# First products of the second MLP moved to the output's banks, P2 ahead of P6, and the last unit taken by halves

## What is computed

```python
x = attention(q, k, v)                 # 2 x 768 tokens, 8 heads of 64; local window and block means
# first MLP, 512 -> 1536 -> 512
rms = sqrt(mean(x * x, axis=-1) + 1e-6)
xn = x / rms * rms_g
g = xn @ w_gate
x = (g * sigmoid(g) * (xn @ w_val)) @ w_out
# second MLP, 512 -> 2048 -> 512
h = x @ w_in2
out = (h - tanh(h)) @ w_out2
```

## Time and profile before

| | |
|---|---|
| median of 3 runs | 623.73 us (623.37 to 624.0) |
| profiled execution, its own time | 624.17 us |
| its span in the trace | 622.0 us |
| PE busy | 610.6 us (98%) |
| DVE, ACT, POOL busy | 429.9, 323.8, 171.1 us |
| TensorE clock granted | 9 of 10 or more in every slice of the page |

### The profile page before, as it was taken

How to read it: one execution, slowest core, us unless ns; L and a number is a source line. 1 busy time by engine, 2 the same in 40 slices (tenths; PEclk the granted TensorE clock), 3 DMA queues, 4 the chain that set the end, 5 groups by cost and what they waited for, 6 DMA issues and landing times.

```text
span 622.0 us, 10724 instructions
## 1 busy us (share of the span) xinstructions
PE 610.6 (98%) x3990; PEld 569.2 (92%) x3990; DVE 429.9 (69%) x699; ACT 323.8 (52%) x622; POOL 171.1 (28%) x223
## 2 busy tenths in 40 slices
PE   8989999999999999999999999999999999999997
PEld 7669999999999998889898899999999989888986
DVE  4899777766653659877776789999534496666643
ACT  5676545444433337555555567766333275555542
POOL 4675421202110322222220745561200222222200
PEclk9999999999999999999999999999999999999999
DMA  9999722332211303222221342224123032222102
GB/s 255 193 241 221 144 63 66 94 94 41 80 53 51 87 9 89 81 69 68 69 69 34 106 134 69 67 69 122 49 76 94 0 99 73 68 69 69 34 2 101
DMA packets 96186, 53.90 MB, mean 87 GB/s; under 512 B 33736, under 2 KB 90312, under 8 KB 95944
## 3 DMA queue, kind: packets, MB, share of 16 engines
q1 hardware_dynamic: 95704, 52.44, 32.6%
q10 hardware_dynamic: 432, 0.79, 0.3%
HBM read 50.07 MB, written 3.15 MB: 86 GB/s over the span
## 4 chain that ended last, share of the span: by engine, by line
PE 90%; ACT 4%; DVE 3%; POOL 2%; issue 1%; DVEq 0%; POOLq 0%; ACTq 0%
PE bank L938 11%; PE bank L940 11%; PE bank L942 11%; PE bank L881 10%; PE bank L883 10%; PE bank L882 10%; PE bank L1047 7%; PE bank L1046 7%; PE bank L1045 7%; PE bank L845 1%; PE bank L865 1%; PE bank L815 1%; POOL sm L614 1%; ACT kT L1224 1%; PE bank L740 1%
## 5 line engine op out<-in xcount | busy, mean ns | idle before, releaser
L1712 DVE TENSOR_TENSOR h_lo<-pd,h_hi 128x384 fp32r<-128x384 f32 x112 | 71.9, 643 | 28.9 <-ACT h_hi L1438 14.0
L1047 PE MATMUL bank<-y_hi,h_lo 128*128 128x512 f32 x192 | 75.5, 393 | 0.0
L1046 PE MATMUL bank<-y_lo,h_hi 128*128 128x512 f32 x192 | 75.4, 393 | 0.0
L1045 PE MATMUL bank<-y_hi,h_hi 128*128 128x512 f32 x192 | 75.3, 392 | 0.0
L704 POOL TENSOR_TENSOR ws_raw<-x_raw 128x256 f32<-128x256 f32 x16 | 11.9, 746 | 209.2 <-PE bank L942 127.6
L881 PE MATMUL bank<-h_hi,z_hi 128*128 128x384 f32 x192 | 64.9, 338 | 0.0
L883 PE MATMUL bank<-h_hi,z_lo 128*128 128x384 f32 x192 | 64.5, 336 | 0.0
L882 PE MATMUL bank<-h_lo,z_hi 128*128 128x384 f32 x192 | 64.5, 336 | 0.0
L1305 ACT CAST h_hi<-pd 128x384 fp32r<-128x384 f32 x48 | 24.7, 515 | 45.5 <-DVE pd L1742 33.5
L1422 ACT COPY part<-bank 128x384 f32<-128x384 f32 x48 | 22.9, 478 | 43.4 <-PE bank L942 42.2
L1047 PEld LDWEIGHTS bank<-y_hi,h_lo 128*128 128x128 f32 x192 | 36.0, 188 | 8.2
(11 more groups left out here) (207 smaller groups left out, 1721.9 us busy)
## 6 DMA issues: line engine op xcount, KB each, us to landing
x_raw<-in_moe_w_in_dram SPq DMA_DIRECT2D x32, 256.0 KB, 3.3
y_raw<-in_moe_w_out_dram SPq DMA_DIRECT2D x32, 256.0 KB, 2.8
x_raw<-in_moe_w_gate_dram SPq DMA_DIRECT2D x24, 256.0 KB, 3.2
y_raw<-in_moe_w_val_dram SPq DMA_DIRECT2D x24, 256.0 KB, 3.3
z_raw<-in_moe_w_out_dram SPq DMA_DIRECT2D x16, 384.0 KB, 3.3
k_rows<-in_k_dram SPq DMA_DIRECT2D x8, 384.0 KB, 5.7
qn<-in_q_dram SPq DMA_DIRECT2D x12, 256.0 KB, 6.6
vw_early<-in_v_dram SPq DMA_DIRECT2D x12, 192.0 KB, 6.3
```

The source lines that it names most:

```text
L1045: nc.tensor.matmul(AB[t][:], a_hi, w_hi, start=begins, stop=False, skip_group_check=True)
L1046: nc.tensor.matmul(AB[t][:], a_hi, w_lo, start=False, stop=False, skip_group_check=True)
L1047: last = nc.tensor.matmul(AB[t][:], a_lo, w_hi, start=False, stop=ends, skip_group_check=True)
L1712: nc.vector.tensor_tensor(dst, full, high.bitcast(f32), ALU.subtract).then_inc(done, 1)
```

## The change

`first_pair` gets banks of its own, all among the six of the output: P1, P6, P7, P4 in bank 7 (`UB0`), P5 in bank 4 (`VB0`, as before), P2 in bank 5 (`WB0`), P3 in bank 6 (`ZB0`). The waits follow: P1 of the next pair no longer waits for the difference of C21, nor its P2 for the sum C12, and the units that begin banks 4 to 7 wait for the readers of those banks instead. P3 no longer waits for the sum C11. `ORDER0`, and the code with it, has the second row of P2 ahead of the second row of P6.

The last unit of all is taken by halves of its columns: DVE first copies the right half of bank 7 (all but the last unit's share) to `stage` (`tail_kept`); PE adds the left half to bank 7 and computes the right half alone into bank 0, three matmuls of 256 columns each; DVE copies the left half and adds bank 0 to the kept right half.

```diff
-        UB, VB, VB0 = bank[0][:, 0:NB], bank[1][:, 0:NB], bank[4][:, 0:NB]
+        UB, VB = bank[0][:, 0:NB], bank[1][:, 0:NB]
+
+        UB0, VB0, WB0, ZB0 = bank[7][:, 0:NB], bank[4][:, 0:NB], bank[5][:, 0:NB], bank[6][:, 0:NB]
...
-        ORDER0 = ("P1", "P5", "P6", "P2", "P7", "P3", "P4")
+        ORDER0 = ("P1", "P5", "P2", "P6", "P7", "P3", "P4")
...
+        def chain_bank(p):
+            return UB if p % NP else UB0
...
                 if begins and t == 2:
-                    pe.wait_ge(total_done, total_no(p, "C12a"))
+                    pe.wait_ge(total_done, total_no(p, "C22"))
+                if begins and t == 3:
+                    pe.wait_ge(total_done, total_no(p, "C11"))
+                if begins and t == 4:
+                    pe.wait_ge(total_done, total_no(p, "C12"))
+                if begins and t == 5:
+                    pe.wait_ge(diff_done, tile_no(p, "C21"))
...
+                if p == G * NP - 1 and k == len(UNITS) - 1:
+
+                    half = DM // 2
+                    pe.wait_ge(diff_done, tile_no(p, "C21"))
+                    pe.wait_ge(tail_kept, 1)
+                    nc.tensor.matmul(AB[t][:, 0:half], a_hi, w_hi[:, 0:half], start=False, stop=False,
+                                     skip_group_check=True)
...
+                    nc.tensor.matmul(bank[0][:, 0:half], a_hi, w_hi[:, half:DM], start=True, stop=False)
...
             def first_pair(g):
                 p = g * NP
                 pe.wait_ge(x_lo_done, pair_weight(p, 0) + 1)
-                pe.wait_ge(x2_dve, x2_dve_no(g, 3))
-                quarter(UB, *operands(p, "P1"), start=True).then_inc(quarter_mm, 1)
-                pe.wait_ge(ws_lo_done, p + 1)
+                pe.wait_ge(x2_dve, x2_dve_no(g, KH))
                 if g:
                     pe.wait_ge(out_act, TT // 2)
                     pe.wait_ge(out_dve, TT // 2)
                 else:
                     pe.wait_ge(xT_lo_done, NT)
+                quarter(UB0, *operands(p, "P1"), start=True).then_inc(quarter_mm, 1)
+                pe.wait_ge(ws_lo_done, p + 1)
                 quarter(VB0, *operands(p, "P5"), start=True).then_inc(quarter_mm, 1)
-                quarter(VB, *operands(p, "P2"), start=True, rows=(0,))
+                pe.wait_ge(x2_dve, x2_dve_no(g, KC - 1))
+                quarter(WB0, *operands(p, "P2"), start=True, rows=(0,))
                 pe.wait_ge(part_done, 3 * p + 1)
-                quarter(UB, *operands(p, "P6"), rows=(0,))
-                pe.wait_ge(x2_dve, x2_dve_no(g, 3) + 5)
-                quarter(UB, *operands(p, "P6"), rows=(1,)).then_inc(quarter_mm, 1)
-                quarter(VB, *operands(p, "P2"), rows=(1,)).then_inc(quarter_mm, 1)
-                pe.wait_ge(x2_dve, x2_dve_no(g, 3) + 6)
+                quarter(UB0, *operands(p, "P6"), rows=(0,))
+                pe.wait_ge(x2_dve, x2_dve_no(g, KC - 1) + 1)
+                quarter(WB0, *operands(p, "P2"), rows=(1,)).then_inc(quarter_mm, 1)
+                pe.wait_ge(x2_dve, x2_dve_no(g, KC - 1) + 5)
+                quarter(UB0, *operands(p, "P6"), rows=(1,)).then_inc(quarter_mm, 1)
+                pe.wait_ge(x2_dve, x2_dve_no(g, KC - 1) + 6)
                 pe.wait_ge(part_done, 3 * p + 2)
-                quarter(UB, *operands(p, "P7")).then_inc(quarter_mm, 1)
+                quarter(UB0, *operands(p, "P7")).then_inc(quarter_mm, 1)
...
-                pe.wait_ge(total_done, total_no(p, "C11"))
-                quarter(VB, *operands(p, "P3"), start=True).then_inc(quarter_mm, 1)
+                quarter(ZB0, *operands(p, "P3"), start=True).then_inc(quarter_mm, 1)
...
             def next_pair(g, i):
...
-                pe.wait_ge(diff_done, tile_no(p - 1, "C21"))
+                if i > 1:
+                    pe.wait_ge(diff_done, tile_no(p - 1, "C21"))
                 quarter(UB, *operands(p, "P1"), start=True).then_inc(quarter_mm, 1)
                 units(1 if i == 1 else 2)
-                pe.wait_ge(total_done, total_no(p - 1, "C12"))
+                if i > 1:
+                    pe.wait_ge(total_done, total_no(p - 1, "C12"))
                 quarter(VB, *operands(p, "P2"), start=True).then_inc(quarter_mm, 1)
...
+                    if g + 1 == G and t == TT - 3:
+
+                        nc.vector.tensor_copy(stage[:, TT - 1, DM // 2:DM],
+                                              AB[TT - 1][:, DM // 2:DM]).then_inc(tail_kept, 1)
...
-                        for c0 in (0, DM // 2):
-                            nc.vector.tensor_copy(stage[:, t, c0:c0 + DM // 2],
-                                                  AB[t][:, c0:c0 + DM // 2]).then_inc(out_dve, 1)
+                        half = DM // 2
+                        nc.vector.tensor_copy(stage[:, t, 0:half], AB[t][:, 0:half]).then_inc(out_dve, 1)
+                        dve.wait_ge(tail_kept, 1)
+                        dve.wait_ge(w2_mm, NP * (g + 1))
+                        nc.vector.tensor_tensor(stage[:, t, half:DM], stage[:, t, half:DM], bank[0][:, 0:half],
+                                                ALU.add).then_inc(out_dve, 1)
```

More of the change, by code:

```diff
@@ L1044, in down_unit @@
                 a_hi, a_lo = h2_hi[:, s, row, b, c0:c0 + P], h2_lo[:, s, row, b, c0:c0 + P]
+                if p == G * NP - 1 and k == len(UNITS) - 1:
[4 more added lines that the diff above has]
+                                     skip_group_check=True)
+                    nc.tensor.matmul(AB[t][:, 0:half], a_hi, w_lo[:, 0:half], start=False, stop=False,
+                                     skip_group_check=True)
+                    nc.tensor.matmul(AB[t][:, 0:half], a_lo, w_hi[:, 0:half], start=False, stop=True,
+                                     skip_group_check=True).then_inc(acc_mm, 1)
+                    nc.tensor.matmul(bank[0][:, 0:half], a_hi, w_hi[:, half:DM], start=True, stop=False)
+                    nc.tensor.matmul(bank[0][:, 0:half], a_hi, w_lo[:, half:DM], start=False, stop=False)
+                    nc.tensor.matmul(bank[0][:, 0:half], a_lo, w_hi[:, half:DM], start=False,
+                                     stop=True).then_inc(w2_mm, 1)
+                    return
                 nc.tensor.matmul(AB[t][:], a_hi, w_hi, start=begins, stop=False, skip_group_check=True)
@@ L1421, in keep_part @@
                 act.wait_ge(quarter_mm, quarter_no(p, product))
-                nc.scalar.copy(part[:, k, :], UB).then_inc(part_done, 1)
+                nc.scalar.copy(part[:, k, :], chain_bank(p)).then_inc(part_done, 1)
             def tanh_tile(p, name):
@@ L1427, in tanh_tile @@
                     act.wait_ge(quarter_mm, quarter_no(p, "P4"))
-                    src = UB
+                    src = chain_bank(p)
                 else:
@@ L1911, in diff_tile @@
                 no = tile_no(p, name) - 1
-                src = UB if name == "C21" else total[:, TOTALS.index(name), :]
+                src = chain_bank(p) if name == "C21" else total[:, TOTALS.index(name), :]
                 dve.wait_ge(tanh2_done, no + 1)
@@ L1926, in first_pair @@
                 x2_bottom(g, KC - 1)
-                add_total(p, "C11", "P2", 3 * p + 1, part[:, 0, :], VB)
+                add_total(p, "C11", "P2", 3 * p + 1, part[:, 0, :], WB0)
                 add_total(p, "C12a", "P5", 3 * p + 2, part[:, 1, :], VB0)
@@ L1933, in first_pair @@
                 dve.wait_ge(total_done, total_no(p, "C12a"))
-                add_total(p, "C12", "P3", 3 * p + 2, total[:, TOTALS.index("C12"), :], VB)
+                add_total(p, "C12", "P3", 3 * p + 2, total[:, TOTALS.index("C12"), :], ZB0)
                 diff_tile(p, "C22")
@@ L2129, in _ @@
                         split_up_sums(0, GATE)
-                    if t < TT - 1:
+                    if g + 1 < G and t == TT - 1:
+                        dve.wait_ge(w2_mm, NP * (g + 1))
+                    else:
                         dve.wait_ge(acc_mm, (TT - 1) * g + t + 1)
-                    else:
-                        dve.wait_ge(w2_mm, NP * (g + 1))
                     if g:
                         dve.wait_ge(out_sent, 16 * TT * g)
+                    if g + 1 == G and t == TT - 3:
+                        nc.vector.tensor_copy(stage[:, TT - 1, DM // 2:DM],
+                                              AB[TT - 1][:, DM // 2:DM]).then_inc(tail_kept, 1)
                     if g + 1 < G or t < TT - 1:
```

9 lines of the change are left out of this document (5 added, 4 removed).

## The result

The changed kernel takes **625.21 us** (median of 10 runs, 624.4 to 626.66); the kernel before, run beside it, 623.94 (10 runs, 623.34 to 624.47). The ratio is 1.0017, with a 95% interval of 1.0009 to 1.0025: 1.06 us longer, between 0.56 and 1.56 (the two medians as they stand lie 1.27 apart). That is surely slower. By the 0.2% of the prediction it counts as no change, but only just: the interval reaches beyond 0.2%. The profiled execution took 625.03 us with a span of 623.3.

The account below looks back on a forecast made before the run. PE was taken as the bound, busy 610.6 of 622.0 us. Group 0 0.53, group 1 0.07 and the end 0.34 sum to 0.94 us; the 623.73 median becomes 624.67, say 624.7 us, range 623.4 to 625.4.

Parts of the forecast that it names:

- last issue: At the kernel's end, the last output DMA is issued at 619.41 in place of 619.54, 0.13 us earlier.
- Stall 1: PE's wait ahead of P7 for ACT's copy of P6, 0.30 us; the new order costs 0.53 us in each group.
- Stall 2: PE's wait ahead of P1 of pair 1 for C21's difference; the new banks gain 0.46 us there in each group.
- the chain: From ACT's copy of P7 through DVE, POOL and `x_sums` to P3 of pair 1; group 0 ends 0.53 us later.
- Group 1: No `x_sums` there and room in the chain, 0.47 us left at P6 of pair 1; 0.07 us later.
- the rival in which group 1 pays in full: P6 of pair 1 waits for `ws_lo` in group 1 too; sum 1.40 us, 625.1 us; chance 0.17.
- The rival in which the banks pay in both groups: P3's wait belongs to something PE leads, so group 0 keeps its 0.46 us; sum 0.48, 624.2 us; chance 0.12.
- the one in which the order costs nothing: The copy of P6 comes earlier and P7 stays at 232.59; sum -0.12 us, 623.6 us; chance 0.08.
- the one in which both stalls go: Both stalls gone in both groups and 0.13 us gained at the end; -1.79 us, 621.9 us; chance 0.03.
- The end: The final 768 KB burst starts with bank 5's DMA, delayed by the new copy; the end comes 0.34 us later.
- the rival drawn from it: The end goes by the last DMA's issue, 0.13 us earlier; sum 0.47 us, 624.2 us; chance 0.18.
- nobody on the path waits for the sum C11: First pair: the swap's earlier C11 gains nothing, since ACT must copy P6 before C11's tanh in either order.

Follow-up runs that it names:

- experiment 1: The kernel before with only the order changed: P2's second row ahead of P6's, old banks, old end; 625.24 us.
- experiment 2: The changed kernel with the old order and the old end, so only the banks and their waits differ from the kernel before; 623.76 us.
- experiment 10: As experiment 7, but in the order P1, P2, P6, P5, P7, so that P5 covers the copy of P6; 622.52 us.
- experiment 5: As experiment 2, and in pair 1 of group 0 DVE makes C22's sum ahead of `x_sums`; 622.91 us.
- experiment 7: Experiments 5 and 6 together: new banks, all of P6 ahead of all of P2, `x_sums` behind C22's sum in pair 1, old end; 622.44 us.
- experiment 4: The kernel before with the last unit by halves, DVE keeping bank 7's right half early, ahead of its wait for bank 5; 624.06 us.
- experiment 9: Experiment 8's unit order, with the last unit by halves and the early kept copy of experiment 4; 623.92 us.
- experiment 6: The kernel before with both rows of P6 ahead of both rows of P2, old banks, old end; 623.96 us.
- experiment 8: The kernel before with the last pair's units reordered so that bank 5 is final two units earlier; 624.04 us.

## Why the prediction was right

The forecast was 624.7 with a range up to 625.4, and 625.21 lies in it, on the side of slower; 0.94 us was the sum, 0.79 is what the distances show (0.89 without the step of 0.10) and 1.06 (0.56 to 1.56) the runs. Of the 0.5 us between 624.7 and 625.21, 0.21 is the kernel before itself, whose median was 623.94 and not 623.73.

| term | forecast | measured |
|---|---|---|
| P7 after the matmul before it | 1.01 | 1.00 in both groups |
| P1 of pair 1: gap | none | none |
| P3 of pair 1, group 0: stall | 0.66 | 0.63 |
| group 0, to P3 of pair 1 | +0.53 | +0.52 (whole group +0.42) |
| group 1 | +0.07 | +0.10, and 0.09 of the end's wait |
| the end | +0.34 | +0.34 to the last byte, +0.27 by the span |
| last issue | 0.13 earlier | 0.10 earlier |

- **Stall 1.** Shown by experiment 1: the order costs 0.52 at P7 in each group, and the gaps at P1 and P3 keep their size. The advice of the Trainium skill (Perfetto Trace Analysis, Optimizing Tensor Performance) to rotate independent groups over banks so that evacuations overlap agrees with experiments 2 and 10, 0.42 us in group 1 by the banks and no gap at P7 once P5 stands between; the changed kernel goes against it in its order.
- **Stall 2 and the chain.** Shown by experiments 2 and 5: the banks' gain comes back at P3 in group 0, and stays as soon as `x_sums` stand behind the sum. That the rest of the chain (low parts, weight load, POOL's sums) follows P7 is seen in the shift of all its rows, 0.52 to 0.54; it was not taken apart further. The prediction missed one stall of PE, the 0.21 at P4 of pair 2 in group 0 (experiment 7). It cost the forecast nothing, since it moved along with the rest: P4 starts 0.36 after its neighbour in the changed kernel too.
- **Group 1.** The margin at P6 of pair 1 was 0.49 (0.47 foreseen), so the rival in which group 1 pays in full is out. The rival in which the banks pay in both groups falls by experiment 2, the one in which the order costs nothing by experiment 1, and the one in which both stalls go by both.
- **The end.** The mechanism held, by experiments 4 and 9: the last issue moves by 0.27 and the end stays. The size, 0.34, is what the last bytes show; by the spans, which are given to 0.1 us, it is 0.27. Whether the 0.07 between them is that rounding or lies behind the last byte is open. The view of landings in the changed kernel (size, time from issue to landing):

```profile
out_dram<-stage SPq DMA_DIRECT2D x1, 256.0 KB, 2.1
out_dram<-stage ACTq DMA_DIRECT2D x1, 256.0 KB, 2.5
out_dram<-stage SPq DMA_DIRECT2D x2, 128.0 KB, 2.5
```

The halves take 0.4 us longer than the bank 5 issued ahead of them, though they have half its bytes, and 0.5 longer than the same halves before. A time that goes by the size alone does not give this; a wait behind the stores ahead of them does. The split in the Trainium skill (DMA: Bandwidth & Descriptors, Anatomy of one DMA) into a fixed time and the bytes over a rate is given there for DMAs that GpSimd issues. These stores are issued by SP and ACT, and when they are queued the split does not hold for them; the rival drawn from it falls by experiments 4 and 9.

**The step that was weak** is the sentence that nobody on the path waits for the sum C11. It was right for this change, as P7's delay hides that chain, but not as a statement of the kernel: experiment 6 ran into that chain once P7 was 0.37 earlier, and lost 0.19 at the first unit. It misled me in the experiments, where I expected the whole of P7's gap from an order that leaves P2's end where it was, and so twice forecast too much (6 and 7).

What stays open: the 0.07 at the end, and the causes of the start's scatter and of the step of 0.10, which were measured and not traced further.

## What to carry to other kernels

When a product is added on top of one that must first be copied out, count the independent matmuls between the two: here three (0.53 us) leave 0.30 open and six close it, and a reordering that takes them away costs their whole length. Before a stall is removed, follow the chain through the other engines to the next place where PE meets it; if an operation on it can be put behind the awaited one, the two edits together pay (0.80 in group 0) where the first alone pays almost nothing (0.07); the second alone was not run. And at the end of a kernel with several output DMAs close together, bring the first of the burst forward, not the last; here that was worth 0.19 us by the trace (experiment 8).

## What was not expected of the hardware

- After a wait on a semaphore the second matmul follows later too: 0.25 in place of 0.175 us behind P7 (233.62 to 233.87), 0.28 behind P3. A stall of PE costs some 0.07 to 0.10 more than its gap.
- Matmuls of 256 columns follow each other after 0.12 us (619.15 to 619.27), in line with 0.175 for 384 and 0.2275 for 512: 0.053 more for each 128 columns, and some 0.015 fixed.
- From PE's last matmul over an ACT copy of 384 columns (0.48) back to PE's next matmul it is 1.00 us, in the changed kernel and in experiment 1, in both groups.
- The program's first 10 us scatter enough to move the rest of the trace by up to 1.5 us, more than any term of this change. For effects of this size, distances within the trace tell more than spans, once a step such as the 0.10 in group 0 has been told apart.
